# Linear attention, routed experts and a dense layer on one core: the first expert's later weight pieces load behind the last chunk, and the token list is built in four parts

## What is computed

```
for t in range(S):                                   # 4 batches x 8 heads, S = 768, D = 64
    state = gamma * state + outer(k[t], v[t])
    y[t] = q[t] @ state / sqrt(D)
x = y, heads side by side                            # 3072 tokens x 512
logits = x @ w_gate + modality_bias[modality_id]     # 8 experts
e = argmax(logits);  gate = softmax(logits)[e]
x = gate * (relu(x @ w1[e]) @ w2[e])                 # 512 -> 1024 -> 512, one expert a token
h = x @ w_in;  out = (h * sigmoid(1.702 h)) @ w_out  # 512 -> 2048 -> 512
```

## Time and profile before

| | |
|---|---|
| median of 3 runs | 924.68 us (923.95 to 927.39) |
| the profiled execution | 926.23 us, of which 924.4 us span |
| PE busy | 907.7 us, 98% of the span |
| DVE, ACT, POOL busy | 58%, 43%, 23% |
| chunks and first expert's load | 0 to 109 us |
| first two tiles and routing tables | 109 to 146 us |
| expert tiles, then the dense layer | 146 us to the end |

### The profile page before, as it was taken

The page is one execution under the profiler, slowest core; times in us unless marked ns, Lnnn a source line. Parts: engine busy times, 40 slices in busy tenths (PEclk is TensorE's granted clock), DMA queues, the critical chain, the costliest instruction groups (busy, mean ns, idle before and its releaser), DMA issues.

```text
span 924.4 us, 18558 instructions
## 1 busy us (share of the span) xinstructions
PE 907.7 (98%) x6709; PEld 787.1 (85%) x6710; DVE 540.3 (58%) x861; ACT 394.4 (43%) x645; POOL 217.2 (23%) x231
## 2 busy tenths in 40 slices
PE   7989999999999999999999999999999999999998
PEld 5777788888888888887888899988899998889997
DVE  3677784555555552233645888544588854567663
ACT  1334423444444442233445554345555434454432
POOL 4635148532115814100120000232000021000003
PEclk9999999999999999999999999999999999999999
DMA  9999677998778866212575655687565567566553
GB/s 345 349 365 409 178 177 247 342 321 271 243 251 280 302 243 200 51 47 71 166 240 175 212 183 185 205 277 237 163 213 183 183 217 236 184 198 209 185 182 139
DMA packets 97216, 204.93 MB, mean 222 GB/s; under 512 B 7676, under 2 KB 50852, under 8 KB 97140
## 3 DMA queue, kind: packets, MB, share of 16 engines
q1 hardware_dynamic: 71056, 128.49, 42.5%
q10 hardware_dynamic: 19188, 55.64, 16.6%
q0 software_dynamic: 6896, 19.77, 7.0%
HBM read 148.00 MB, written 55.88 MB: 221 GB/s over the span
## 4 chain that ended last, share of the span: by engine, by line
PE 96%; issue 1%; DMA 1%; POOL 1%; DVE 0%; another core or an unknown queue 0%; ACT 0%; POOLq 0%; SPq 0%
PE bank L2005 27%; PE bank L2007 27%; PE bank L2006 27%; PE bank L2044 2%; PE bank L1911 2%; PE bank L1882 2%; PE bank L1931 1%; PE bank L1864 1%; PE bank L1920 1%; PE bank L2122 1%; PE bank L1898 1%; DMA kv_in<-kv 1%; PE bank L1945 1%; PE bank L1952 0%
## 5 line engine op out<-in xcount | busy, mean ns | idle before, releaser
L2005 PE MATMUL bank<-ring,act_hi 128*128 128x256 f32 x672 | 190.5, 283 | 0.0
L2006 PE MATMUL bank<-ring,act_hi 128*128 128x256 f32 x672 | 190.2, 283 | 0.0
L2007 PE MATMUL bank<-ring,act_lo 128*128 128x256 f32 x672 | 190.2, 283 | 0.0
L866 ACT ACTIVATE act_hi<-act_f 128x1024 fp32r<-128x1024 f32 x84 | 89.0, 1059 | 117.6 <-PE bank L2007 117.6
L2005 PE MATMUL bank<-mix_hi,ring 128*128 128x512 f32 x336 | 131.5, 391 | 0.0
L2007 PE MATMUL bank<-mix_hi,ring 128*128 128x512 f32 x336 | 130.8, 389 | 0.0
L2006 PE MATMUL bank<-mix_lo,ring 128*128 128x512 f32 x336 | 130.7, 389 | 0.0
L2005 PEld LDWEIGHTS bank<-ring,act_hi 128*128 128x128 f32 x672 | 129.0, 192 | 0.5
L1718 DVE TENSOR_TENSOR act_lo<-act_f,act_hi 128x1024 fp32r<-128x1024 f32 x84 | 102.8, 1223 | 45.3 <-ACT act_hi L866 45.1
L2006 PEld LDWEIGHTS bank<-ring,act_hi 128*128 128x128 f32 x672 | 129.0, 192 | 0.1
L2007 PEld LDWEIGHTS bank<-ring,act_lo 128*128 128x128 f32 x672 | 129.0, 192 | 0.0
(11 more groups left out here) (246 smaller groups left out, 1507.6 us busy)
## 6 DMA issues: line engine op xcount, KB each, us to landing
ring<-w_parts SPq DMA_DIRECT2D x84, 512.0 KB, 4.6
ring<-w_parts SPq DMA_DIRECT2D x24, 1024.0 KB, 5.8
ring<-w_parts SPq DMA_DIRECT2D x24, 768.0 KB, 4.8
w_parts<-part_hi ACTq DMA_DIRECT2D x16, 896.0 KB
qk_in<-qk SPq DMA_DIRECT2D x24, 512.0 KB, 7.4
raw<-w SPq DMA_DIRECT2D x24, 512.0 KB, 6.1
kv_in<-kv SPq DMA_DIRECT2D x20, 512.0 KB, 8.6
mix_in<-w_quads ACTq DMA_DIRECT2D x16, 512.0 KB
```

The source lines that it names most:

```text
L866: copy = lambda dst, src: nc.scalar.activation(dst, src, ACT.Copy)
L2005: mm(dst, hi, w_hi, start=first, stop=False, skip_group_check=skip)
L2006: mm(dst, hi, w_lo, start=False, stop=False, skip_group_check=skip)
L2007: return mm(dst, lo, w_hi, start=False, stop=last, skip_group_check=skip)
```

## The change

It has five parts.

1. The first four pieces of the first expert are loaded with chunks 15 to 18 and no longer with chunks 13 to 16. Pieces 4 to 7 are loaded behind the last chunk's own loads, and no longer with chunks 19 to 22.
2. The splits follow: the high and low part of piece 0 in chunk 17, of 1 in 18, of 2 in 19, of 3 in 20, of 4 in 21, of 5 in 22, of 6 and 7 in 23. DVE's small steps `order_early`, `size_early` and `take_early` move from chunks 18 and 21 to chunks 15 and 16.
3. The early gathers of POOL move from chunk 16 to chunk 22.
4. The token list's 24 matmuls are written as four parts of six. The first part stands ahead of the last quarter of the first tile's `down`, the others behind it, and the turn of the second tile's hidden rows follows them.
5. The gathers of tiles 2 to 4 read the columns of `token_of_slot` itself, without the copy. SP waits for the first of them to land before it loads the next expert's pieces.

```diff
-EARLY_LOAD_AT = 13
-EARLY_PIECES_AT = {EARLY_LOAD_AT: (0,), 14: (1,), 15: (2,), 16: (3,), 19: (4,), 20: (5,), 21: (6,), 22: (7,)}
-EARLY_SPLIT_AT = {14: 0, 15: 1, 16: 2, 17: 3, 19: 4, 20: 5, 22: 6, 23: 7}
...
+EARLY_LOAD_AT = 15
+EARLY_PIECES_AT = {15: (0,), 16: (1,), 17: (2,), 18: (3,), TILES - 1: (4, 5, 6, 7)}
+EARLY_SPLIT_AT = {17: (0,), 18: (1,), 19: (2,), 20: (3,), 21: (4,), 22: (5,), TILES - 1: (6, 7)}
+COUNT_AT, CHOOSE_AT, PLACE_AT, LIST_AT, ORDER_AT = EARLY + 1, EARLY + 2, EARLY + 5, EARLY + 8, EARLY + 9
+EARLY_GATHER_AT = TILES - 2
...
             n_used = steering(sp, T_NUSED, 1, NE)
+            sp.wait_ge(xg_in[EARLY_TILES], DMA_INC)
...
-            pool.wait_ge(token_ready, 1)
...
-                hold(slot_idx_ready, tile + (1 - EARLY_TILES))
...
+                hold(slot_idx_ready, tile + (1 - XG_BUFS))
+                gather_x(buf, slot_idx[:, buf:buf + 1])
...
+            hold(token_ready, 1)
             for k in range(EARLY_TILES, XG_BUFS):
-                gather_slots(k, k)
+                gather_x(k, token_of_slot[:, k:k + 1])
...
-                if t == ORDER_AT + TRIPLE:
+                if t == ORDER_AT + 1:
                     size_early()
                     take_early()
...
-            down(0, 0, at_slot, 0, ps_y_of[0], False)
...
+            def list_tokens(nth):
+
+                n = TILES // HOT_PARTS
+                pe.wait_ge(tile_tok_ready, nth * TILE_PARTS // HOT_PARTS + 1)
+                pe.wait_ge(onehots_ready, nth + 1)
+                for t in range(nth * n, (nth + 1) * n):
+                    last = mm(ps_token, lane_hot[:, t, :], tile_tok[:, t, :], start=(t == 0), stop=(t == TILES - 1))
+                if nth == HOT_PARTS - 1:
+                    last.then_inc(token_done, 1)
+
+            down(0, 0, at_slot, 0, ps_y_of[0], False, (0, 1, 2))
+            list_tokens(0)
+            down(0, 0, at_slot, 0, ps_y_of[0], False, (3,))
+            for nth in range(1, HOT_PARTS):
+                list_tokens(nth)
             turn_hidden(1, 0)
-            for t in range(TILES):
...
-            last.then_inc(token_done, 1)
```

More of the change, by code:

```diff
@@ L156 @@
 swapped = lambda pair: pair % 2 == 1
-EARLY_LOAD_AT = 13
-EARLY_PIECES_AT = {EARLY_LOAD_AT: (0,), 14: (1,), 15: (2,), 16: (3,), 19: (4,), 20: (5,), 21: (6,), 22: (7,)}
-EARLY_SPLIT_AT = {14: 0, 15: 1, 16: 2, 17: 3, 19: 4, 20: 5, 22: 6, 23: 7}
-assert len(EARLY_SPLIT_AT) == EXPERT_PIECES
-COUNT_AT, CHOOSE_AT, PLACE_AT, LIST_AT, ORDER_AT = EARLY + 1, EARLY + 2, EARLY + 5, EARLY + 8, EARLY + 12
-EARLY_GATHER_AT = LIST_AT + 2
+EARLY_LOAD_AT = 15
[3 more added lines that the diff above has]
+EARLY_GATHER_AT = TILES - 2
 EARLY_MARK = 8
@@ L709, in _, with gather_x @@
                 gather_gate(tile, token_of_early[:, tile:tile + 1], early_gates_in)
-            pool.wait_ge(token_ready, 1)
             for s in x_stored:
                 pool.wait_ge(s, DMA_INC * TILES // 2)
+            def gather_x(buf, tokens):
+                pool.indirect_dma_start(out=xg[:, buf, :], out_offset=None, in_=x_rows,
+                                        in_offset=bass.IndirectOffsetOnAxis(ap=tokens, axis=0)).then_inc(xg_in[buf], DMA_INC)
             def gather_slots(tile, buf):
                 nc.gpsimd.tensor_copy(slot_idx[:, buf:buf + 1], token_of_slot[:, bass.ds(tile, 1)]).then_inc(slot_idx_ready, 1)
-                hold(slot_idx_ready, tile + (1 - EARLY_TILES))
-                pool.indirect_dma_start(out=xg[:, buf, :], out_offset=None, in_=x_rows,
-                                        in_offset=bass.IndirectOffsetOnAxis(ap=slot_idx[:, buf:buf + 1], axis=0)).then_inc(
-                    xg_in[buf], DMA_INC)
+                hold(slot_idx_ready, tile + (1 - XG_BUFS))
+                gather_x(buf, slot_idx[:, buf:buf + 1])
             def split_pieces(rank, place, before):
@@ L900, in _ @@
                     store_x(t - 2)
-                if t in EARLY_SPLIT_AT:
-                    first_hi(EARLY_SPLIT_AT[t])
+                for i in EARLY_SPLIT_AT.get(t, ()):
+                    first_hi(i)
             copy_xT(TILES - 1)
@@ L1432, in _ @@
                     order_early()
-                if t == ORDER_AT + TRIPLE:
+                if t == ORDER_AT + 1:
                     size_early()
                     take_early()
-                if t in EARLY_SPLIT_AT:
-                    first_lo(EARLY_SPLIT_AT[t])
+                for i in EARLY_SPLIT_AT.get(t, ()):
+                    first_lo(i)
             x_lo(0)
@@ L2064, in _ @@
             turn(ps_gate, gate[:, :], identity).then_inc(gateT_done, 1)
-            down(0, 0, at_slot, 0, ps_y_of[0], False)
-            turn_hidden(1, 0)
-            for t in range(TILES):
[L2068 to L2072, removed]
-                last = mm(ps_token, lane_hot[:, t, :], tile_tok[:, t, :], start=(t == 0), stop=(t == TILES - 1))
-            last.then_inc(token_done, 1)
+            def list_tokens(nth):
[11 more added lines that the diff above has]
+                list_tokens(nth)
+            turn_hidden(1, 0)
             down(0, 0, at_slot, 1, ps_y_of[0], False)
```

## The result

The changed kernel took 927.54 us (median of 21 runs, 923.25 to 934.25); the kernel before, measured beside it, 925.03 (21 runs). The ratio is 1.0025, interval 1.0013 to 1.0037: slower by 1.2 to 3.4 us. The forecast was 924.7 with a range up to 927.2, so the time lies outside it, on the side of the loss.

The account below looks back on a forecast made before the run. PE, busy 907.7 of 924.4 us, was taken to bound the kernel. From the profiled 926.2, - 1.1 (long chunks) + 1.1 (double split) + 0 left 926.2, so the median stayed at 924.7; range 921.2 to 927.2.

Parts of the forecast that it names:

- Two splits in chunk 23: End of the chunk stage: a second high part on ACT makes PE begin 1.1 us later, bounds 0.9 and 1.3.
- The pieces out of the queue: Pieces 4 to 7 loaded behind the chunk loads: long chunks 19 and 20 shorten, saving 1.1 us, bounds 0 and 1.1.
- 0 of 2.9 in chunks 14 to 16: Pieces 0 to 3 loaded two chunks later: none of the 2.9 us in these long chunks is saved.
- the 0.31: Excess of the step into chunk 19, 4.03 against an undisturbed 3.72 us, counted as savable.
- The first rival: Chunk stage: full queues do not cause the long chunks, so only the 1.1 us cost is left: 925.8 us, chance 0.20.
- The rival of ACT held in chunk 21: ACT waits 0.9 us for piece 4, with the copy PE needs behind it: 926.7 us or more, chance 0.12.
- The case of all going well: All 4.0 us of long chunks and the 1.65 us of lower clock vanish, less the cost: 920.1 us, chance 0.08.
- about 1 as a sign: Sign for the forecast: `outputs` of chunk 23 starts about 1 us sooner, at 103.5.
- The token list: Moving six narrow matmuls forward saves 0; the lower-clock window behind the list could save up to 1.65 us.
- a sign against my forecast: Behind the token list: a granted clock of 1.00 would show the forecast wrong.
- gathers by columns and SP's wait: Hand-over to the next experts: POOL comes forward 2.9 us and SP's loads wait until about 133 us, both priced zero.
- within 0.5%: Whole kernel: the measured time stays within 0.5% (4.6 us), too little to tell from no change, chance 0.88.

Follow-up runs that it names:

- e1: The changed kernel without SP's wait for the gather ahead of the next expert's loads: 926.08 us, ratio 1.0017 to the kernel before.
- e2: The chunk half alone: kernel before with parts 1 to 3 of the change, old token list, gathers and SP loads: 924.21 us, ratio 0.9984.
- e4: The changed kernel with piece 6 split in chunk 22, so chunk 23 has one split: 927.26 us, ratio 1.0020 to the kernel before.
- e8: Kernel before with parts 1 to 3 of the change, but piece 6 split in chunk 22: 923.89 us, ratio 0.9990.
- e16: The changed kernel with a copy and wait ahead of each of three gate gathers, 1.96 us apart: 925.47 us, ratio 1.0002 to the kernel before.
- e11: The changed kernel with the old gathers of tiles 2 to 5 (copy, then gather), SP's wait kept: 925.26 us, ratio 1.0004 to the kernel before.
- e5: Kernel before with only SP's wait for the gather of tile 2 added: 925.63 us, ratio 1.0006.
- e18: The changed kernel itself measured once more: 926.20 us, ratio 1.0016 to the kernel before.
- e3: Kernel before with parts 4 and 5 of the change alone (list in four parts, column gathers, SP's wait): 928.45 us, ratio 1.0030.
- e13: Kernel before with column gathers alone, POOL's wait for the token list at its old place: 925.95 us, ratio 1.0013.

## Why the prediction was wrong, step by step

**The sum held up to the token list.** *Two splits in chunk 23*, + 1.1 with bounds of 0.9 to 1.3: the waits are 1.06 us in the profile after, and the stretch is longer by 0.8 us, a little under the lower bound. The way there was right (two high parts ahead of the last copy, PE waiting for ACT and then DVE); 0.3 of it was caught up by steps that no longer waited.

**The pieces out of the queue**, - 1.1 in the long chunks 19 and 20, and 0 of 2.9 in chunks 14 to 16. The distance from chunk 12 to chunk 23 is 44.0 to 45.8 us (mean 45.1) in the 11 profiles with the old loads and 42.5 to 44.7 (mean 43.4) in the nine with the new: - 1.7 us. By chunk, in the means: into 20, 4.24 to 3.44 (- 0.8, as forecast); into 19, 4.79 to 4.62 (- 0.2; the 4.03 of the earlier trace rows was the one short step of its kind, so the 0.31 was read off an exception); into 14, 4.42 to 3.85, and into 15, 5.78 to 5.45 (- 0.9 together, forecast as 0). Into 21 it is longer, 4.54 to 4.88: PE has a hole by "issue" there of up to 1.3 us in five of the nine (e1, e2, e4, e8, e16), while the last pieces keep the queues full (DMA share 1.04 at the hole of e8). The forecast had leaned on a chunk 21 without a hole; 4.18 was the shortest such step of before's order, and pieces 4 to 7 fill just that stretch. The forecast was right in kind and under by 0.6. With the double split the stage comes to - 0.9; the chunk half alone measured - 0.9 by the medians, - 0.6 to - 2.4 by the ratio.

The cause is less sure than the size. The first rival's number (only the cost is left) has fallen, since the steps did get shorter; its mechanism, that the full queues are not the cause, has not. But the DMA share stayed at 1.00 to 1.04 in the profile after, from 62 to 78 us as from 88 to 96, while the steps into 14 and 20 lost their holes. Parts 1 to 3 of the change also move splits of ACT and DVE out of chunks 14 to 16, DVE's small steps and POOL's early gathers, and no run moves the loads alone. What makes a hole by "issue" stays open. The rival of ACT held in chunk 21 has fallen: ACT's idle time ahead of every high part there is its usual 0.40 us. The case of all going well had the right sign for chunks 14 and 15, with a third of its size.

In the two profiles of before and after this gain doesn't show (43.3 against 44.0, less the split): 44.0 is the shortest of the eleven. And `outputs` of chunk 23 did start 1.65 us sooner, where I had named about 1 as a sign; 0.95 of that was there at chunk 12 already (59.64 for 60.59), ahead of any edit. The sign was right for a reason that wasn't mine.

**The token list**, 0 with a bound of - 1.65 for the clock. In the profile after the clock is 1.00 there, which I had named as a sign against my forecast. No gain shows in the medians. The rows of before were one profile of the eleven with the old order of the list, and only four of these have the stretch. A term that rests on a clock event in one profile should carry a chance, not a length.

**The step that failed is the last term: gathers by columns and SP's wait, "Zero" and "Zero".** It held two errors.

SP's wait was priced by who *needs* the loads: "queued behind it are only those, and POOL splits them after 142". That is true, and POOL never waited for them. It left out whom the loads *meet*. 2 MB moved from 124 to 132 us, where the loads met only POOL's first gathers, for which PE didn't wait, to 138 to 150 us, among ACT's quads, the gathers and the stores to `y_slots`, on which `y_out` and then PE wait. The trace of before had the warning: `y_out` at 150.30 already waited 1.21 us for `y_slots` there, without PE noticing. How much more it could bear, the runs show: waits of 2.44 and 2.56 us (e16, e11) still cost PE nothing, 2.71 (e5) cost 0.30, 2.93 (e18) 0.79, and 3.37 to 4.23 (after, e4, e3) 0.99 to 1.85. SP's wait is worth about 0.5 us alone, and PE waits 0.8 to 1.9 us for `y_out` in four of the five kernels that hold both edits (none in e16). The loads also came late, at 137.9 for the 133 that I had put; without the crawl they start at 132.5 to 133.5 in the kernels with the new chunks (e11, e16, e18), so that number was right for an execution without it.

The column gathers were priced by what POOL gains (2.9 us, and POOL is indeed ahead: its third gather at 131.78 for 134.22) and by who waits for POOL (nobody). What a denser row of indirect transfers does to the others was not asked. The old copy with its wait, 1.0 us of POOL for each, looked like pure overhead; no kernel that kept it had a late signal. No row of before showed six in a row, so the term needed a bound on the side of a loss, and had none. By the medians it cost 1.1 to 2.1 us in the changed kernel (+ 0.4 with the old gathers, against + 2.5 and + 1.5 in its two measurements).

**The rivals:** none had its place. The slower one had the sign and nearly the size (926.7), with another mechanism; its microsecond isn't where the loss was. The chances: "within 0.5%" holds, since 2.5 us is 0.27%.

## What to carry to other kernels

A load that is moved later is not free because its user can wait: look at what else is in the queues at its new time, above all at stores whose landing frees a buffer, and at how much each of these already waits beneath the cover of another engine.

An engine that is ahead of everyone gains nothing from being faster, and making it issue more densely can cost the others, as it did here in 6 of 9 profiles. Where an edit gives only to an engine with slack, its price should be bounded on the side of a loss.

One profile of each kernel is one draw, and so is one measurement. Distances between fixed marks, taken over all profiles of a study, separated 0.8 us cleanly where medians with intervals of 2 us did not. And where a cost comes in some executions only, the number of long runs says more than the median: 20 of 110 above 929 us against 1 of 115.

## What the runs showed of the hardware that I had not expected

- While POOL issued six indirect transfers 1.25 us apart (0.95 us each and 0.30 between), and for some 4 us behind them, most of SP's register instructions took 0.69 to 0.72 us instead of 0.02 to 0.28, and a signal of PE reached ACT 2.4 us late (3.7 in another kernel). With pauses of one more 0.7 us ahead of three of the six it did not occur, in one profile of each of two kernels.
- The same kernel (columns alone) gave 931.16 us in one measurement and 925.14 in another, 6 us apart, while the kernel before stayed within 0.2 (925.19 and 925.40). The two measurements were on two chips; each of the two has profiles with a late signal and profiles without.
- A gap of 3.29 us on PE was followed by 3.4 us at the lower clock, and so cost 5 us (columns alone), while gaps of 1.92 to 1.95 us in three kernels (after, e4 and e13) were not.
- Two high parts in a row ahead of PE's last chunk: 0.79 to 0.86 us, the same within 0.1 us in all six profiles that have them.
